# Weights split one step later in the attention, their last part loaded and split behind it, and one chunk of scores in other banks

## The chip, the cores and the metric

The kernel runs on one core of one Trainium2 chip. The time is device microseconds of one execution; the median of three is given, with the lowest and the highest. The engines are PE (TensorE, matrix products and transposes, writing to PSUM banks), ACT (ScalarE), DVE (VectorE), POOL (GpSimd) and SP (SyncE, which here only issues DMAs). Each engine works through its own instructions in the order written; between engines there are only semaphores.

## The reference

Three parts follow each other, all in float32:

```
attention  q, k, v: [4 batches, 8 heads, 576 rows, 64]
           scores = q k^T / 8, masked where 64-row block i < block j
           probs  = exp(scores - max) / (sum + 1e-9);  attn = probs v
           x = attn, heads side by side: [2304 tokens, 512]
first net  h = x w_in [512, 2048]; g = max(h, 0) + log1p(exp(-|h|)); y = g w_out [2048, 512]
experts    tokens with y w_skip > 0: expert = argmax(y w_gate) of 8,
           out = y + weight * (relu(y w1[e]) w2[e]);  other tokens: out = y
```

## The kernel before

**Attention** (`attention`, called first in each engine's program). The 32 (batch, head) pairs are taken two at a time: 16 pairs p of heads. For each p the 576 rows of scores come in five chunks i = 0 to 4 of 128 rows (the last of 64). PE multiplies a chunk (`score`, L333 and L339) into PSUM, DVE masks it and takes its negative maximum (`two_maxima` for chunks 0 and 1, `maximum` for the others), ACT takes the exponential and the sum (`exponent`, L459), DVE forms the inverse of the sums (`invert`, L574 and L575; once for chunks 0 to 2, once for 3 and 4), POOL multiplies probs by it (`scale`, L269), PE turns probs (`turn_probs`, L352, units named p0, p1, p2a, p2b, p3a, p3b, p4, p4end), ACT and DVE copy what is turned out of PSUM, and PE multiplies with v (`mix_left` L364, `mix_right` L376). The turns of probs and the mixtures of pair p are written in step p+1, between the scores of pair p+1. PE also turns q and k of the next pair (`turn_qk`: units q, k, ends; L319, L313), and DVE copies them to qT and kT (`copy_qk`).

**Banks.** PSUM has eight banks: four for scores, two for `turned`, two for `mixed`. `score_tile` gives chunks 0, 1 and 3 of a pair banks 0 and 1 of scores, chunks 2 and 4 banks 2 and 3. `score` therefore waits on the semaphore `probs_ready`, which ACT raises after each chunk's exponentials: chunk 3 for chunks 0 and 1 of its pair, chunk 4 for chunk 2, chunk 0 of the next pair for chunk 3, chunk 2 of the next pair for chunk 4. The two `turned` banks alternate: each unit waits for the copy of the unit before the last. The mixtures' first use of `mixed` is `mix_left(0)`, in step 1.

**Weights.** w_in and w_out are kept in two parts each, a rounded `high` and the remainder `low`, and every product is made of three. The split is done while the attention runs: 16 parts w of 128x1024, eight of w_in and eight of w_out. SP loads part w to one of two halves of `stage` (`load_weights`), and POOL makes high (a cast, L280) and low (a subtraction, L282) in `split(w)`. In POOL's order, step p (0 to 15) is: the scalings of chunks 3 and 4 of pair p-1, then `split(p)`, then the scalings of chunks 0 to 2 of pair p. SP loads parts 0 and 1 ahead of its loop and part p+1 in its round p, behind the loads of q, k and v of later pairs; a load waits until the part that was in its half of stage is split.

**The blocks** (`rest`). The 2304 tokens are taken in six blocks of 384, and the loop over n has its own body for the first and the last. In each block there are 16 hidden chunks f (L999 to L1001: x by columns of w_in) and 16 product rows (`rows_chunk`, L1010 to L1012: g by rows f of w_out), three chunks behind; the softplus between them is ACT's (L1221 to L1227) and DVE's (L1405 to L1411). Product rows 13 to 15 of a block lie in the round of the next block. Then ACT copies the finished rows to `y` (`copy_rows`), SP stores y, and POOL sorts rows to the experts. Hidden chunks 0 to 2 of block 0 are written between the last turns and mixtures of the attention. `x_parts`, `mag`, `u` and others of this part lie where `stage` and q and k of the attention were, and `y` where the attention's `probsT` is; so DVE's third and fourth split of x (`split_x(2)`, `split_x(3)`) wait for weights_split 15 and ACT's first softplus for 16. Last come the experts, whose weights are loaded at the end of the blocks.

The change touches `score_tile` and `score` (PE's waits and banks), SP's loop in `sync`, POOL's loop in `gpsimd`, the wait in `vector`, and in `rest` SP's, POOL's, PE's (`rows_chunk`) and ACT's (`copy_rows`) programs.

Of the kernel before, what the change touches and what calls it, by code (L numbers as in the profile page):

```python
# [25 lines left out]
P = 128  # L26
# [41 lines left out]
def build(nc, q, k, v, w_in, w_out, w_skip, w_gate, w1, w2, out):  # L68
    B, H, S, D = q.shape
    DM, FF = w_in.shape  # L70
    E, _, EF = w1.shape
    N = B * S
    PAIRS = B * H // 2
    JP = H // 2
    CH = (S + P - 1) // P
    FULL = S // P
    TAIL = S - FULL * P
    assert D == 64 and DM == H * D == 4 * P and TAIL == 64 and CH == 5
    SCALE = 1.0 / 8.0
    assert SCALE * SCALE * D == 1.0  # L80

    x_heads = nc.dram_tensor("x_heads", (DM, N), F32).ap()


    x_sorted = nc.dram_tensor("x_sorted", (E * (N + ROUND) + ROUND, DM + 2), F32).ap()

    qf, kf, vf = (t.rearrange("b h s d -> (b h) s d") for t in (q, k, v))

    whole = ExitStack()

    def sem(name, into=whole):
        return into.enter_context(nc.semaphore(name))

    def sb(into, name, shape, dtype=F32):
        return into.enter_context(nc.sbuf_tensor(name, shape, dtype))

    def ps(into, name, shape):
        return into.enter_context(nc.psum_tensor(name, shape, F32))

    with whole:  # L100
        ident = sb(whole, "ident", [P, P])
        with ExitStack() as feed:

            win = {p: sb(feed, f"w_in_{p}", [P, DM // P, FF], F32R) for p in ("high", "low")}
            wout = {p: sb(feed, f"w_out_{p}", [P, FF // P, DM], F32R) for p in ("high", "low")}
            x_raw = sb(feed, "x_raw", [P, DM // P, TILES * P])
            router = sb(feed, "router", [P, DM // P, GROUP])
            x_stored = sem("x_stored")
            attended = attention(nc, qf, kf, vf, w_in, w_out, w_gate, w_skip, x_heads, ident, win, wout, x_raw, router,
                                 x_stored, sem, sb, ps, (B, H, S, D, PAIRS, JP, CH, FULL, TAIL, SCALE, DM, FF, E))  # L110
            rest(nc, x_heads, x_sorted, out, w1, w2, ident, win, wout, x_raw, router,
                 x_stored, PAIRS, attended, feed, sem, sb, ps, (N, DM, FF, E, EF))


def attention(nc, qf, kf, vf, w_in, w_out, w_gate, w_skip, x_heads, ident, win, wout, x_raw, router,
# [3 lines left out]
    with own:  # L119
# [41 lines left out]
        SPLIT = 2 * P  # L161

# [21 lines left out]
        def score_tile(p, i):  # L186

            if i < 2:
                return scores[:, 0:2, ROW[i]:ROW[i] + P * (i + 1)]
            b = 2 if i % 2 == 0 else 0  # L190
            return scores[:, b:b + 2, 0:P * (i + 1)] if i < FULL else scores[:, b:b + 2, 0:S // 2]

        def sync(sp):
# [44 lines left out]
            load_weights(0)  # L238
            load_weights(1)
            for p in range(PAIRS + 2):  # L240
# [3 lines left out]
                if 1 < p < PAIRS:  # L244
                    load_v(p)
                if 0 < p < PAIRS - 1:
                    load_weights(p + 1)
                if p > 1:
# [12 lines left out]
        def gpsimd(pool):  # L261
# [22 lines left out]
            for p in range(PAIRS + 1):  # L284
                if p > 0:
                    pool.wait_ge(s["inverse_ready"], 2 * p)
                    for two in range(2):
                        scale(3, two)
                    scale(FULL, 0)
                if p < PAIRS:  # L290
                    split(p)
                    pool.wait_ge(s["inverse_ready"], 2 * p + 1)
# [4 lines left out]
        def tensor(pe):  # L297
# [25 lines left out]
            def score(p, i):  # L323
                if i == 0:
                    pe.wait_ge(s["copied_by_vector"], copies[p - 1, "ends"][1])

                if i != 1 and CH * p + i > 2:
                    pe.wait_ge(s["probs_ready"], CH * p + (-1, None, 0, 2, 3)[i])
                tile = score_tile(p, i)
# [210 lines left out]
        def vector(dve, split_x):  # L540
# [88 lines left out]

            dve.wait_ge(s["weights_split"], PAIRS - 1)  # L630
            split_x(2)
# [12 lines left out]

def rest(nc, x_heads, x_sorted, out, w1, w2, ident, win, wout, x_raw, router,
         x_stored, PAIRS, attended, feed, sem, sb, ps, sizes):
# [84 lines left out]
    counted = parts[0:1, 0:E * MOST[0]].rearrange("p (e m) -> p e m", e=E)  # L731

    hidden = ps(feed, "hidden", [P, 2, BANK])
    rows_out = ps(feed, "rows_out", [P, TILES, DM])
# [11 lines left out]
             "exps_ready", "chosen_ready", "ranks_ready", "slots_ready", "sorted",  # L746
             "tally_ready", "blank", "closed", "closed_by_pool", "parts_ready", "parts_copied", "constants_ready", "vector_steps", "constant_steps", "waited")
    s = {n: sem("b_" + n) for n in names}
# [41 lines left out]
    with late:  # L790
# [32 lines left out]
        def _(sp):  # L823
# [6 lines left out]
            def store_rows(n):  # L830
                sp.wait_ge(s["rows_copied"], TILES * (n + 1))
                sp.dma_start(out[bass.ds(n * T, T), :].rearrange("(t p) d -> p t d", p=P), y[:, :, 0:DM])\
                  .then_inc(s["rows_stored"], 16)

            sp.wait_ge(x_stored, 16 * PAIRS)
            sp.wait_ge(s["x_ready"], K)
# [76 lines left out]
        def _(pool):  # L913
# [28 lines left out]
                           allow_small_or_imprecise_dtypes=True).then_inc(s["constants_ready"], 1)  # L942

            def sort(n):

# [39 lines left out]
        def _(pe):  # L985
# [27 lines left out]

            def rows_chunk(n, f):
                pe.wait_ge(s["g_ready"], F * n + f + 1)
                for t in range(TILES):
# [198 lines left out]
        def _(act):  # L1215
# [19 lines left out]
            def copy_rows(n, t):  # L1235
                if t == 0:
                    act.wait_ge(x_stored, 16 * PAIRS)
                    need(act, s["rows_stored"], 16 * n)
                    need(act, s["sorted"], 16 * TILES * n)
# [41 lines left out]

            act.wait_ge(att["weights_split"], PAIRS)
            chunk(0, 0)
# [391 lines left out]
```

## Time and profile before

| | |
|---|---|
| median of 3 runs | 700.47 us (699.14 to 701.51) |
| the profiled execution | 700.94 us |
| its span, first to last instruction | 699.3 us |
| mean granted clock of PE | 0.991 of full |
| PE busy | 676.8 us (97%) |
| PE's weight loads busy | 521.2 us (75%) |
| DVE, ACT, POOL busy | 433.3 us (62%), 404.5 us (58%), 165.4 us (24%) |
| chain that ended last | PE 86%, DVE 4%, DMA 2%, issue 2%, SP's queue 2%, ACT 1%, POOL 1% |

All times below are microseconds from the span's start. The attention lasts until about 211, the blocks until about 640, the experts to the end. A row of the timeline gives the start, how long it took, the engine, the line, the operation and its tiles (out<-in), the count of like instructions merged into the row, and in brackets how long the engine was idle before it and who released it. Successive matmuls overlap at their ends, so the start of the next row says better than a row's length how long PE was held. The granted clock is given as a share of full speed: 1.00 is 2.4 GHz, 0.50 is 1.2 GHz.

### The profile page before, as it was taken

The numbers are of one execution on the slowest core, as the hardware profiler recorded it, in microseconds if no ns is written. First come the engines' busy times: TensorE is split into PE (matmuls) and PEld (weight loads), VectorE is DVE, ScalarE is ACT, GpSimd is POOL, SyncE is SP. The second block draws the span as 40 slices with busy tenths as digits, with TensorE's granted clock in tenths as the row PEclk, the third lists the DMA queues.
The fourth block names the chain that finished last, engine by engine and source line by source line (L and its number), as shares of the span: only waits on it lengthen the run. The fifth ranks groups of instructions, "written<-read, shape, count | busy, mean of one in ns | idle before, by whom it ended". The sixth has DMA issues, their size and how long they took to land.

```text
span 699.3 us, 12929 instructions
## 1 busy us (share of the span) xinstructions
PE 676.8 (97%) x3990; PEld 521.2 (75%) x3990; DVE 433.3 (62%) x1049; ACT 404.5 (58%) x990; POOL 165.4 (24%) x227
## 2 busy tenths in 40 slices
PE   6999999999999999999999999999999999999895
PEld 4565555656578999889989998899888988864342
DVE  5566676767666676567656765676567656746122
ACT  3576666667775566656565656565656565542221
POOL 2767767676741000001000200020002000103111
PEclk9899999999999999999999999999999999999998
DMA  8355665554202000200020002000200010079170
GB/s 202 92 154 140 174 169 144 148 138 125 83 35 70 1 1 1 92 0 12 0 90 0 9 0 90 0 0 0 90 0 12 0 45 0 3 260 357 52 257 25
DMA packets 79439, 53.73 MB, mean 77 GB/s; under 512 B 61192, under 2 KB 64264, under 8 KB 79392
## 3 DMA queue, kind: packets, MB, share of 16 engines
q1 hardware_dynamic: 75952, 50.60, 24.1%
q0 software_dynamic: 1920, 1.73, 0.9%
q10 hardware_dynamic: 1520, 0.82, 0.4%
q8 instruction: 24, 0.39, 0.2%
q14 instruction: 23, 0.19, 0.1%
HBM read 41.18 MB, written 16.28 MB: 82 GB/s over the span
## 4 chain that ended last, share of the span: by engine, by line
PE 86%; DVE 4%; DMA 2%; issue 2%; SPq 2%; ACT 1%; POOL 1%; DVEq 0%; ACTq 0%; POOLq 0%
PE hidden L999 9%; PE hidden L1001 9%; PE hidden L1000 9%; PE rows_out L1012 9%; PE rows_out L1010 9%; PE rows_out L1011 9%; PE turned L352 8%; PE scores L333 6%; PE mixed L376 5%; PE scores L339 2%; PE hidden L1113 2%; PE rows_out L1128 2%; PE mixed L364 2%; DMA softplus_done<-x_sorted 1%; PE turned_y L1037 1%
## 5 line engine op out<-in xcount | busy, mean ns | idle before, releaser
L1221 ACT ACTIVATE mag<-hidden 128x384 f32<-128x384 f32 x96 | 47.3, 492 | 151.6 <-PE hidden L1001 149.8
L999 PE MATMUL hidden<-x_parts,w_in_high 128*128 (+1 forms) x384 | 132.8, 346 | 0.5 <-DVEq L1413 0.4
L1001 PE MATMUL hidden<-x_parts,w_in_low 128*128 (+1 forms) x384 | 129.4, 337 | 0.0
L1000 PE MATMUL hidden<-x_parts,w_in_high 128*128 (+1 forms) x384 | 129.4, 337 | 0.0
L948 POOL DMA_INDIRECT x_sorted<-y,slot x18 | 20.5, 1140 | 406.7 <-DVE slot L1462 403.1
L1012 PE MATMUL rows_out<-w_out_high,g_low 128*128 128x512 f32 x288 | 114.0, 396 | 0.0
L1010 PE MATMUL rows_out<-w_out_high,g_high 128*128 128x512 f32 x288 | 113.7, 395 | 0.4 <-DVE g_low L1420 0.4
L1011 PE MATMUL rows_out<-w_out_low,g_high 128*128 128x512 f32 x288 | 113.5, 394 | 0.0
L459 ACT ACTIVATE probs<-scores,neg_max 128x128 f32<-128x128 f32 (+3 forms) x128 | 67.1, 530 | 21.7 <-DVE neg_max L554 15.1
L269 POOL TENSOR_SCALAR probs<-probs,inverse 128x128 f32<-128x128 f32 (+3 forms) x128 | 66.9, 544 | 52.6 <-DVE inverse L575 52.6
L999 PEld LDWEIGHTS hidden<-x_parts,w_in_high 128*128 128x128 f32 x384 | 72.1, 188 | 8.3 <-issue 3.1
L1420 DVE TENSOR_TENSOR g_low<-g,g_high 128x384 fp32r<-128x384 f32 x96 | 53.6, 558 | 36.4 <-DVE g L1411 34.3
L1000 PEld LDWEIGHTS hidden<-x_parts,w_in_high 128*128 128x128 f32 x384 | 72.2, 188 | 2.2
L1001 PEld LDWEIGHTS hidden<-x_parts,w_in_low 128*128 128x128 f32 x384 | 72.1, 188 | 0.0
L1405 DVE TENSOR_SCALAR small<-u 128x384 uint32<-128x384 f32 x96 | 34.8, 362 | 59.0 <-ACT u L1223 57.8
L1410 DVE COPY_PREDICATED log<-small,series 128x384 f32<-128x384 uint32 x96 | 58.1, 605 | 17.3 <-DVE series L1407 17.3
L1012 PEld LDWEIGHTS rows_out<-w_out_high,g_low 128*128 128x128 f32 x288 | 54.1, 188 | 12.5
L352 PEld LDWEIGHTS turned<-ident,probs 128*128 128x128 f32 x320 | 34.3, 143 | 36.9 <-issue 27.5
L1010 PEld LDWEIGHTS rows_out<-w_out_high,g_high 128*128 128x128 f32 x288 | 54.1, 188 | 9.5 <-DVE g_low L1420 1.1
L1011 PEld LDWEIGHTS rows_out<-w_out_low,g_high 128*128 128x128 f32 x288 | 54.1, 188 | 8.7
L352 PE MATMUL turned<-ident,probs 128*128 128x128 f32 x320 | 53.1, 290 | 5.2 <-ACT probsT L468 3.2
L1407 DVE SCALAR_TENSOR_TENSOR series<-square,u 128x384 f32<-128x384 f32 x96 | 53.3, 555 | 4.5
(179 smaller groups left out, 1058.0 us busy)
## 6 DMA issues: line engine op xcount, KB each, us to landing
whole_w<-in_moe_w_dram SPq DMA_DIRECT2D x12, 1024.0 KB, 11.3
x_heads<-x_pair SPq DMA_DIRECT2D x16, 288.0 KB, 2.1
x_raw<-x_heads SPq DMA_DIRECT2D x6, 768.0 KB, 5.6
out_dram<-y SPq DMA_DIRECT2D x6, 768.0 KB, 4.0
q_nat<-in_q_dram SPq DMA_DIRECT2D x32, 128.0 KB, 2.6
v_nat<-in_v_dram SPq DMA_DIRECT2D x32, 128.0 KB, 2.4
stage<-in_moe_w_in_dram SPq DMA_DIRECT2D x8, 512.0 KB, 3.9
stage<-in_moe_w_out_dram SPq DMA_DIRECT2D x8, 512.0 KB, 3.7
```

The lines of the kernel that those rows point to most:

```text
L269: nc.gpsimd.tensor_scalar(to, to, inverse[:, i, two:two + 1], 1.0, ALU.mult, ALU.mult)\
L352: last = nc.tensor.transpose(to[0:kr, n * P:n * P + P], rows[:, P * c:P * c + kr], ident[:])
L459: last = nc.scalar.activation(to, scored, ACT.Exp, bias=neg_max[:, i, two:two + 1], accum_out=sums[:, i, two:two + 1])
L999: nc.tensor.matmul(o, win["high"][:, k, cols], high, start=(k == 0), stop=False)
L1000: nc.tensor.matmul(o, win["high"][:, k, cols], low, start=False, stop=False)
L1001: last = nc.tensor.matmul(o, win["low"][:, k, cols], high, start=False, stop=(k == K - 1))
L1010: nc.tensor.matmul(o, high, wout["high"][:, f, :], start=(f == 0), stop=False)
L1011: nc.tensor.matmul(o, high, wout["low"][:, f, :], start=False, stop=False)
L1012: return nc.tensor.matmul(o, low, wout["high"][:, f, :], start=False, stop=(f == F - 1))
L1407: step.then(nc.vector.scalar_tensor_tensor(series[:], square[:, b, :], REST, u[:, b, :], ALU.add, ALU.mult))
L1410: step.then(nc.vector.copy_predicated(log[:, b, :], small[:], series[:]))
L1420: nc.vector.tensor_tensor(g_low[f % RING][:], g[:, f % 2, :], g_high[f % RING][:], ALU.subtract)\
```

## The change

There are two edits.

1. **Part w is split in step w+1.** POOL's step 0 has no split; step p has `split(p-1)` for p from 1 to 15. SP loads only part 0 ahead of its loop and part p in round p, for p from 1 to 14. Part 15, the last two rows f of w_out (14 and 15), is not split in the attention: behind the last mixture SP loads it to the place of `y`, POOL splits it behind its constants, PE waits for that ahead of product row 14 of each block but the last (a wait that is written in the loop), and ACT ahead of each block's first copy to y. DVE's x_parts 2 and 3 still wait for 15 splits, which is now the split made in step 15; ACT's first softplus waits for 15 in place of 16.
2. **The fourth chunk of scores of pair 0** goes to the two banks of `mixed` and waits for nothing; chunk 0 of pair 1 then waits only for the exponentials of chunks 0 and 1 of pair 0.

```diff
+        LAST_PART = PAIRS - 1
@@ score_tile
+            if p == 0 and i == 3:
+                return mixed[:, :, 0:P * (i + 1)]
             b = 2 if i % 2 == 0 else 0
@@ sync
             load_weights(0)
-            load_weights(1)
             for p in range(PAIRS + 2):
...
-                if 0 < p < PAIRS - 1:
-                    load_weights(p + 1)
+                if 0 < p < LAST_PART:
+                    load_weights(p)
@@ gpsimd
                     scale(FULL, 0)
+                    if p <= LAST_PART:
+                        split(p - 1)
                 if p < PAIRS:
-                    split(p)
                     pool.wait_ge(s["inverse_ready"], 2 * p + 1)
@@ score
-                if i != 1 and CH * p + i > 2:
-                    pe.wait_ge(s["probs_ready"], CH * p + (-1, None, 0, 2, 3)[i])
+                if i != 1 and CH * p + i > 2 and (p, i) != (0, 3):
+                    pe.wait_ge(s["probs_ready"], CH * p + (-1 if p > 1 else -3, None, 0, 2, 3)[i])
@@ vector
-            dve.wait_ge(s["weights_split"], PAIRS - 1)
+            dve.wait_ge(s["weights_split"], LAST_PART)
@@ rest
+    last_part = y[:].rearrange("p t d -> p (t d)")[:, 0:2 * DM]
+    LAST_F = 2 * (PAIRS - 1 - PAIRS // 2)
@@ rest, sync
+            sp.wait_ge(att["mixed_right_ready"], PAIRS)
+            sp.dma_start(last_part.rearrange("p (f n) -> p f n", n=DM),
+                         w_out[LAST_F * P:(LAST_F + 2) * P, :].rearrange("(f p) n -> p f n", p=P))\
+              .then_inc(s["last_part_loaded"], 16)
             sp.wait_ge(x_stored, 16 * PAIRS)
@@ rest, gpsimd, behind the constants
+            pool.wait_ge(s["last_part_loaded"], 16)
+            high, low = (wout[h][:, LAST_F:F, :].rearrange("p f n -> p (f n)") for h in ("high", "low"))
+            nc.gpsimd.tensor_copy(high, last_part).then_inc(s["last_part_high"], 1)
+            pool.wait_ge(s["last_part_high"], 1)
+            nc.gpsimd.tensor_tensor(low, last_part, high, ALU.subtract).then_inc(s["last_part_split"], 1)
@@ rows_chunk
+                if f == LAST_F:
+                    pe.wait_ge(s["last_part_split"], 1)
                 pe.wait_ge(s["g_ready"], F * n + f + 1)
@@ copy_rows
                     act.wait_ge(x_stored, 16 * PAIRS)
+                    act.wait_ge(s["last_part_split"], 1)
@@ scalar of rest
-            act.wait_ge(att["weights_split"], PAIRS)
+            act.wait_ge(att["weights_split"], PAIRS - 1)
```

## Rows read from the trace of the kernel before

**Rows 1.** Busy time in two stretches: length, engines (x instructions), PEclk, DMA share, GB/s
```profile
30.00:60.00 30.00, 29.33 (x223) 17.78 (x222) 19.57 (x51) 20.34 (x64) 21.97 (x32) 1.00 0.53 138
220.00:280.00 60.00, 60.00 (x303) 54.38 (x302) 39.70 (x81) 36.14 (x77) 0.00 (x0) 1.00 0.00 1
```

**Rows 2.** Timeline of PE, steps 0 and 1
```profile
8.93 0.66 PE L319 MATMUL turned<-ident,q_nat 128*128 128x128 f32 x4
11.49 1.13 PE L333 MATMUL scores<-kT,qT 64*128 64x512 f32 x4 [1.90 <-ACT probs L459]
...
13.40 1.19 PE L339 MATMUL scores<-kT,qT 64*64 64x288 f32 x8
15.78 0.93 PE L333 MATMUL scores<-kT,qT 64*128 64x128 f32 x8 [1.19 <-ACT probs L459]
18.41 0.69 PE L352 MATMUL turned<-ident,probs 128*128 128x128 f32 x2 [1.71 <-POOL probs L269]
19.32 1.11 PE L352 MATMUL turned<-ident,probs 128*128 128x128 f32 x4 [0.22 <-POOL probs L269]
...
25.72 0.66 PE L352 MATMUL turned<-ident,probs 128*128 128x128 f32 x4
```

**Rows 3.** Timeline of POOL, split of part 0 and pair 0's scalings
```profile
14.17 1.04 POOL L280 CAST w_in_high<-stage 128x1024 fp32r<-128x1024 f32 x1 [12.48 <-DMA stage<-in_moe_w_in_dram]
15.29 2.34 POOL L282 TENSOR_TENSOR w_in_low<-stage,w_in_high 128x1024 fp32r<-128x1024 f32 x1
17.62 4.10 POOL L269 TENSOR_SCALAR probs<-probs,inverse 128x128 f32<-128x128 f32 x8
```

**Rows 4.** Timeline of DVE, steps 0 and 1
```profile
10.77 0.68 DVE L595 TENSOR_SCALAR qT<-turned 128x512 f32<-128x512 f32 x1
12.72 0.17 DVE L561 MEMSET scores<- 64x128 f32 x1 [1.27 <-PE scores L333]
...
14.07 0.68 DVE L597 COPY kT<-turned 128x512 f32<-128x512 f32 x1
...
15.26 0.19 DVE L575 RECIPROCAL inverse<-sums_eps 128x6 f32<-128x6 f32 x1
```

**Rows 5.** Busy time in three stretches around the fall of the clock
```profile
8.00:12.00 4.00, 2.10 (x14) 1.08 (x12) 2.94 (x7) 2.28 (x11) 0.00 (x0) 1.00 0.77 171
14.00:18.00 4.00, 1.51 (x14) 0.63 (x10) 3.25 (x12) 2.28 (x6) 3.75 (x4) 1.00 1.05 257
18.00:25.00 7.00, 6.37 (x22) 3.86 (x24) 2.78 (x7) 3.17 (x12) 6.92 (x10) 0.52 0.50 125
```

**Rows 6.** Timeline of ACT, end of pair 0's third chunk and copy of p0
```profile
12.34 0.23 ACT L459 ACTIVATION_READ_ACCUMULATOR probs<-scores,neg_max 128x1 f32 x1
...
20.99 0.36 ACT L468 COPY probsT<-turned 128x256 f32<-128x256 f32 x1
```

**Rows 7.** Timeline of PE, third chunk of scores to p3a in step 2
```profile
34.08 0.92 PE L333 MATMUL scores<-kT,qT 64*128 64x384 f32 x4
...
37.64 0.66 PE L352 MATMUL turned<-ident,probs 128*128 128x128 f32 x4
```

**Rows 8.** Issue of q of pair 2 by SP, and its time to landing
```profile
11.28 0.98 SPq L200 DMA_DIRECT2D q_nat<-in_q_dram  x2
...
q_nat<-in_q_dram SPq DMA_DIRECT2D x2, 128.0 KB, 4.5
```

**Rows 9.** Timelines of POOL, DVE and SP at the attention's end
```profile
191.22 2.65 POOL L282 TENSOR_TENSOR w_out_low<-stage,w_out_high 128x1024 fp32r<-128x1024 f32 x1
...
195.60 0.28 DVE L587 COPY probsT<-turned 64x128 f32<-64x128 f32 x1
...
193.34 18.38 SPq L230 DMA_DIRECT2D x_heads<-x_pair  x3
```

**Rows 10.** Timeline of PE, product row 14 of block 0
```profile
271.61 0.39 PE L1010 MATMUL rows_out<-w_out_high,g_high 128*128 128x512 f32 x1
```

**Rows 11.** Waits of PE: total, times, longest
```profile
PE hidden L1113 <- issue: 1.8, 2, 1.3
```

More of the change, by code:

```diff
@@ L110, in build @@
                                  x_stored, sem, sb, ps, (B, H, S, D, PAIRS, JP, CH, FULL, TAIL, SCALE, DM, FF, E))
-            rest(nc, x_heads, x_sorted, out, w1, w2, ident, win, wout, x_raw, router,
+            rest(nc, x_heads, x_sorted, out, w_out, w1, w2, ident, win, wout, x_raw, router,
                  x_stored, PAIRS, attended, feed, sem, sb, ps, (N, DM, FF, E, EF))
@@ L642, in attention, with rest @@
     return sync, gpsimd, tensor, scalar, vector, s, turned_count
-def rest(nc, x_heads, x_sorted, out, w1, w2, ident, win, wout, x_raw, router,
+def rest(nc, x_heads, x_sorted, out, w_out, w1, w2, ident, win, wout, x_raw, router,
          x_stored, PAIRS, attended, feed, sem, sb, ps, sizes):
@@ L731, in rest @@
     counted = parts[0:1, 0:E * MOST[0]].rearrange("p (e m) -> p e m", e=E)
+    last_part = y[:].rearrange("p t d -> p (t d)")[:, 0:2 * DM]
+    LAST_F = 2 * (PAIRS - 1 - PAIRS // 2)
+    assert LAST_F == F - 2
     hidden = ps(feed, "hidden", [P, 2, BANK])
@@ L746, in rest @@
              "exps_ready", "chosen_ready", "ranks_ready", "slots_ready", "sorted",
-             "tally_ready", "blank", "closed", "closed_by_pool", "parts_ready", "parts_copied", "constants_ready", "vector_steps", "constant_steps", "waited")
+             "tally_ready", "blank", "closed", "closed_by_pool", "parts_ready", "parts_copied", "last_part_loaded", "last_part_high", "last_part_split", "constants_ready", "vector_steps", "constant_steps", "waited")
     s = {n: sem("b_" + n) for n in names}
```

## The prediction

> **What bounds the kernel now.** The page's busy shares and its chain of waits (table above) come first: PE is busy nearly throughout and is most of the chain. Then the busy time by stretches: from 30 to 60 us, in the attention, PE works 29.33 of 30 us, from 220 to 280 us, in the blocks, all 60.00 [rows 1]. So a change can win only where PE's queue is thin, and lose only by what it puts into the full part. The thin place is the beginning, and I read PE's instructions there one by one, with POOL, DVE and ACT beside them.
>
> The reader sees three gaps in PE [rows 2]: 1.90 us ahead of pair 0's fourth chunk of scores (11.49), which waits for ACT's exponentials to free its banks; 1.19 us ahead of pair 1's first scores (15.78), the same reason two chunks further; 1.71 us ahead of the first turned probs (18.41), which wait for POOL's scaling. POOL is late because the split of weight part 0 stands ahead of the scalings in its queue: it waits for its load until 14.17 and works until 17.62, though DVE has had the inverse ready at 15.26+0.19 = 15.45 [rows 3, 4]. Behind the gaps the granted clock falls: it is 1.00 (2.4 GHz) over 8-12 and 14-18 us and 0.52 on average over 18-25, which is 1.2 GHz for nearly all of it [rows 5]. Ahead of the fall, in 14-18, PE had been busy 1.51 of 4 us.
>
> **Term 1, the start of the chain.** I walk the new order with the old durations.
> PE: the turn of q of pair 1 begins at 8.93 and takes 0.6 (its row says 0.66, the last matmul overlapping). The fourth chunk goes to mixed's two banks and waits for nobody: 9.5 in place of 11.49, and with 1.1 it ends at 10.6. The turn of k, as long as that of q, ends at 11.2. The turn of the ends needs the bank that DVE empties with qT, 10.77+0.68 = 11.4, and is over by 11.8 [rows 2, 4]. The fifth chunk still waits for the third's exponentials, ACT 12.34+0.23 = 12.57 [rows 6]: 12.6 in place of 13.40. With 1.1 it ends at 13.7.
> DVE: mask and maximum of the fourth chunk took 14.07-12.72 = 1.35 and now begin behind qT at 11.4, to 12.75. kT, the ends and the inverse took 15.45-14.07 = 1.4: the ends are copied by 13.6, the inverse is ready at 14.1 [rows 4]. The masks and maxima work on mixed's banks as they did on those of scores, the same instructions of the same size.
> Pair 1's first scores want only the first two chunks' exponentials (over before 12) and the ends: they start at 13.7, not 15.78.
> POOL: with no split in step 0 it scales when the inverse is there, 14.1 and a semaphore, say 14.2, in place of 17.62. The second turn of probs came 19.32-17.62 = 1.70 behind that start, so now 15.9 [rows 2, 3]. **It is 3.4 us earlier.** What is late next is DVE's inverse; no load stands before it any more.
> Loads that must keep up: q of pair 2 is issued from 11.28 to 12.3 and lands 4.5 later, 16.8 at most [rows 8], and is wanted at 18.0 (below). SP now issues one 512 KB load less ahead of it, so it comes earlier if anything; k of pair 1 stands further ahead still. Part 0's load, there at 14.17, is wanted behind pair 0's scalings, at 14.2+4.10 = 18.3 and later.
>
> **Term 2, the clock.** From the second turn (19.32) to the turn called p3a (25.72) PE took 6.40 us, nearly all at the low rate [rows 2, 5]. At the high rate: the second turn 0.5 (half of its 1.11), to 16.4; from the third chunk to p3a a later step takes 37.64-34.08 = 3.56 [rows 7], which gives 20.0. One wait of that stretch is longer here: the third turn needs ACT's copy of the first, whose end was 20.99+0.36 = 21.35, 2.03 behind the second turn's start [rows 6]; less the 0.5 by which that turn is shorter it is 17.5, and without it the third turn would start at 16.4+0.85 = 17.3. So +0.3: p3a at 20.3, 4.4 us behind the second turn in place of 6.4. **That is 2.0 us more**, if the clock stays high. Low rate remains possible, so I weigh it by the nearest rows. In 8-12 us PE was busy 2.10 of 4 us and the clock was still high in 14-18; in 14-18 it was busy 1.51, and the clock fell [rows 5]. In the new order its gaps are 0.2 at 11.2, 0.8 at 11.8, 0.4 ahead of the first turn of probs, 0.6 between it and the second, 0.3 ahead of the third: no 4 us with less than 2.5 busy. That is nearer to the row that kept the clock. I take 2.0; the ends are 0 and 2.3 (ACT's 0.3 gone too).
> The Trainium skill (TensorE: Matmul & The Clock Gate, "The HAM clock gate") says that how many matmuls run at the low rate differs from run to run of one kernel. One profile of before stands here, so no row shows that; by it some runs of before would lose less than 2.0, and the changed kernel's time would be what the sum gives.
>
> **From p3a on** PE's order is the old one and PE has no slack to swallow the lead [rows 1], so all of it is carried on. A POOL step keeps its scalings and one split, with the part's number one less; each part is loaded one round later and used one later, with the same distance between. Cost 0, hidden by the time POOL had to spare in each step.
> **Step 15.** DVE's x_parts 2 and 3 now wait for a split of this very step. That split (now of part 14) ended at 191.22+2.65 = 193.87; DVE comes there at 195.60+0.28 = 195.8 [rows 9]. Hidden with 1.9 us to spare; without it, what is missing would go to hidden chunk 0's last products one for one.
> **The last part.** SP issues it behind its last store, in whose row the queue is free at 193.34+18.38 = 211.7; at the 4.5 us of the slow group it lands at 216.2 [rows 8, 9]. POOL has its constants first, then cast and subtract, 1.04+2.65 = 3.7 [rows 3, 9]: about 220 by the old clock of the trace. Its first reader is product row 14 of block 0 at 271.61 [rows 10]; some 50 us cover it, and ACT's copy to y, which now waits for it too, is two product rows later. Each queue it is moved past has room: in SP's stand the reload of x_raw for block 1 (used late in block 0) and the padding store, in POOL's the first sort, after block 0. Uncovered it would cost what it lasts beyond that, one for one.
> **Beside DVE.** The split now runs next to DVE's softplus. In step 15, next to busy DVE, POOL's subtract took 2.65 where part 0's took 2.34 [rows 3, 9]: both sides may lose some 0.3 us, and an equal loss on DVE meets products wanted three chunks later. Cost 0; with no cover 0.3 to 0.6.
> The Trainium skill (GPSIMD Engine Reference, "Key points") says that GpSimd shares its SBUF interfaces with VectorE and contends with some of its instructions. The rows agree with 0.31 us; by the rule, were all of it on the path, the sum would be up to 0.6 smaller.
> **Added waits.** PE gets one ahead of product row 14 of five blocks; behind it stand nine products and the next hidden chunk. It is satisfied long before. The nearest row: such waits stand ahead of every chunk in 220-280, and PE has no gap [rows 1]. 0 each. The other end is the longest gap of "issue" ahead of a matmul, 1.3 us in the expert tail [rows 11], far from it in kind. ACT's six stand in an engine with idle time in each chunk.
>
> **Sum.** The profiled execution took 700.94 us, 699.3 span and 1.6 around it. 3.4+2.0 = 5.4 less: 695.5. The median before is 700.47, 0.5 lower, inside the spread of its runs (699.14 to 701.51); that would make it 695.1 by median. I stay with 695.5 and leave the half us to the range.
>
> **Rivals.**
> 1. *The clock falls all the same*, somewhat earlier or later. For: 2.3 us of gaps remain within 5. Against: the denser order, by the two rows above. Only 3.4 is won: 697.5.
> 2. *Another wait in the gap's place*: a load of pair 1 or 2 comes late (or DVE does the inverse where it did), so POOL starts at 15.5, won 2.1 instead of 3.4, and with the longer gaps the clock is lost too: 698.8. For: landings of 4.5 us. Against: 1.2 us to spare at the tightest.
> 3. *Slower: the loop's new wait stalls PE*, at product row 14, five times. From 5.4/5 = 1.1 us each the kernel is slower than before, from 1.5 measurably; if each stall is as long as the longest of PE's gaps above, 1.90 [rows 2], it is 9.5 and the time 705.0. For: gaps of "issue" of 1.3 us exist behind waits of the tail [rows 11]. Against: PE has waits of this kind ahead of every chunk and no gap.
> 4. *It doesn't do what it says*: ACT or POOL sets the pace of a pair, and the lead is given back before the blocks. Against: PE is busy 29.33 of 30 us there. 700.5.
>
> **Chances.** Forecast 62% (its own range 694.2 to 696.4), rival 1 19%, rival 2 9%, rival 3 4%, rival 4 6%. The range, 694.2 to 698.0, holds the forecast and rival 1 with the unknown ends of the clock and of the contention. What a measurement of this kernel can't tell from no change is 0.3%, 2.1 us about 700.47. Faster (under 698.4): forecast, rival 1 and a third of 2, 84%. Same: rival 4 and the rest of 2, 12%. Slower: rival 3, 4%.
>
> **What would show it.** PE: the fourth chunk at 9.5 without a gap, pair 1's first scores at about 13.7, the second turn of probs at 15.9, p3a at 20.3, the clock at 1.00 from 8 to 30 us. POOL: first scaling at 14.2, its first split behind pair 0's scalings. x_parts 2 and 3 without a wait; the last part split some 50 us ahead of product row 14, and no gap there in any block. It is wrong if the clock is 0.50 anywhere from 9 to 30 us, if POOL is idle at 14.2, if DVE waits ahead of the inverse, if a pair takes longer than before, or if PE waits in the blocks.

## The result, and the profile after

| | before | changed |
|---|---|---|
| median | 700.99 us (699.14 to 702.99, 6 runs) | 697.14 us (696.10 to 698.19, 6 runs) |
| ratio, 95% interval | | 0.9942 (0.9922 to 0.9961) |
| profiled execution, span | 700.94, 699.3 us | 697.28, 695.7 us |
| mean granted clock of PE | 0.991 | 0.998 |

The changed kernel is 3.9 us faster by the medians and 3.7 by the two profiled executions; 695.5 was forecast, 5.4 less. The interval of the ratio runs from 2.7 to 5.5 us. (The ratios of this document are worked out apart from the medians and differ from their quotients by up to 0.002, so some gains are given by both.)

PE of the changed kernel, steps 0 and 1 (columns as in [rows 2]):

```profile
8.44 1.57 PE L338 MATMUL scores<-kT,qT 64*128 64x128 f32 x12 [0.46 <-DVE kT L605]
9.94 0.66 PE L324 MATMUL turned<-ident,q_nat 128*128 128x128 f32 x4
10.53 1.13 PE L338 MATMUL mixed<-kT,qT 64*128 64x512 f32 x4
11.59 0.65 PE L324 MATMUL turned<-ident,k_nat 128*128 128x128 f32 x4
...
13.62 1.19 PE L344 MATMUL scores<-kT,qT 64*64 64x288 f32 x8 [0.70 <-ACT probs L464]
14.82 0.93 PE L338 MATMUL scores<-kT,qT 64*128 64x128 f32 x8
15.96 0.44 PE L357 MATMUL turned<-ident,probs 128*128 128x128 f32 x2 [0.21 <-POOL probs L273]
16.87 0.66 PE L357 MATMUL turned<-ident,probs 128*128 128x128 f32 x4 [0.47 <-POOL probs L273]
17.45 0.92 PE L338 MATMUL scores<-kT,qT 64*128 64x384 f32 x4
18.77 0.52 PE L357 MATMUL turned<-ident,probs 128*128 128x128 f32 x3 [0.41 <-ACT probsT L473]
...
21.46 0.66 PE L357 MATMUL turned<-ident,probs 128*128 128x128 f32 x4
```

The three large gaps of [rows 2] are gone. The fourth chunk follows the turn of q with no gap, and p3a comes at 21.46 in place of 25.72: 4.26 us earlier. POOL and DVE of the same stretch:

```profile
15.17 4.09 POOL L273 TENSOR_SCALAR probs<-probs,inverse 128x128 f32<-128x128 f32 x8 [13.49 <-DVE inverse L580]
...
19.94 1.03 POOL L284 CAST w_in_high<-stage 128x1024 fp32r<-128x1024 f32 x1
```

```profile
14.68 0.16 DVE L579 TENSOR_SCALAR sums_eps<-sums 128x6 f32<-128x6 f32 x1
14.88 0.19 DVE L580 RECIPROCAL inverse<-sums_eps 128x6 f32<-128x6 f32 x1
```

POOL scales 0.1 us behind the inverse, and its first split stands behind pair 0's scalings. Against [rows 3] the scalings start 2.45 us earlier. The busy times in the stretches of [rows 5]:

```profile
8.00:12.00 4.00, 3.56 (x24) 2.05 (x24) 2.86 (x10) 1.27 (x7) 0.00 (x0) 1.00 0.75 162
14.00:18.00 4.00, 3.31 (x26) 1.64 (x22) 3.78 (x13) 3.11 (x11) 2.83 (x7) 1.00 0.72 165
18.00:25.00 7.00, 6.37 (x48) 3.78 (x44) 5.07 (x11) 5.33 (x16) 5.32 (x5) 1.00 0.42 124
```

PE is busy the same 6.37 us of the last stretch, but with 48 matmuls in it and not 22: the granted clock is 1.00 there and not 0.52. The last part, and its first reader:

```profile
211.47 1.28 POOL L960 CAST w_out_high<-y 128x1024 fp32r<-128x1024 f32 x1 [0.60 <-DMA y<-in_moe_w_out_dram]
212.84 2.83 POOL L962 TENSOR_TENSOR w_out_low<-y,w_out_high 128x1024 fp32r<-128x1024 f32 x1
```

```profile
267.37 0.39 PE L1030 MATMUL rows_out<-w_out_high,g_high 128*128 128x512 f32 x1
```

It is ready at 215.7 and wanted at 267.37, 51.7 us later. From 20 to 620 us the waits of PE (total, times, longest) are:

```profile
PE turned L357 <- ACT probsT L473: 3.4, 15, 0.3
PE hidden L1019 <- DVEq L1436: 0.5, 1, 0.5
PE rows_out L1030 <- DVE g_low L1443: 0.4, 1, 0.4
```

The kernel before has the same three kinds (3.2, 0.4 and 0.4 us). The last two lie in the last block, which has no wait for the last part: the third is ahead of its product row 14, at 615.46, and waits for DVE's g_low. At product row 14 of the five blocks that do wait for the last part PE has no gap. Comparing matmul by matmul, the lead of 4.26 us at p3a is 4.25 at the end of the attention and 4.33 late in the last block. The tail of experts is 0.7 longer here: from the 3500th of 3990 matmuls to the end of the span took 90.7 us before and 91.4 after.

### The profile page after: what moved, and what is told of

Read it like the earlier page. It is cut to its first block, busy times and chain, and to the rows that moved or that the text cites. A ratio compares the mean times of both kernels' runs of the same rounds, so it can differ in the third digit from the quotient of the medians.

```text
span 695.7 us, 12935 instructions
## 1 busy us (share of the span) xinstructions
PE 675.2 (97%) x3990; PEld 520.5 (75%) x3990; DVE 434.6 (62%) x1049; ACT 404.2 (58%) x990; POOL 165.7 (24%) x227
## 4 chain that ended last, share of the span: by engine, by line
PE 90%; DVE 4%; issue 2%; ACT 2%; DMA 1%; POOL 0%; DVEq 0%; ACTq 0%; POOLq 0%
PE hidden L1019 9%; PE hidden L1021 9%; PE hidden L1020 9%; PE rows_out L1032 9%; PE rows_out L1030 9%; PE rows_out L1031 9%; PE turned L357 8%; PE scores L338 6%; PE mixed L381 5%; PE rows_out L1150 3%; PE hidden L1135 3%; PE scores L344 3%; PE mixed L369 2%; PE turned_y L1059 1%; ACT probsT L473 1%
## 5 line engine op out<-in xcount | busy, mean ns | idle before, releaser
L464 ACT ACTIVATE probs<-scores,neg_max 128x128 f32<-128x128 f32 (+3 forms) x126 | 65.6, 527 | 18.7 <-DVE neg_max L559 16.5
L1433 DVE COPY_PREDICATED log<-small,series 128x384 f32<-128x384 uint32 x96 | 58.2, 607 | 17.3 <-DVE series L1430 17.3
L357 PE MATMUL turned<-ident,probs 128*128 128x128 f32 x320 | 51.7, 285 | 4.5 <-ACT probsT L473 3.9
```

What stands on the lines that cost most here:

```text
L357: last = nc.tensor.transpose(to[0:kr, n * P:n * P + P], rows[:, P * c:P * c + kr], ident[:])
L464: last = nc.scalar.activation(to, scored, ACT.Exp, bias=neg_max[:, i, two:two + 1], accum_out=sums[:, i, two:two + 1])
L1433: step.then(nc.vector.copy_predicated(log[:, b, :], small[:], series[:]))
```

## Experiments

The table has, of every profile, the start of pair 0's first scores, POOL's first scaling and p3a, then p3a behind the first scores and behind the scaling, the stretch from the 100th to the 3500th matmul, and the tail behind it (filler matmuls not counted in the numbering). All are worked out from starts in the traces.

| kernel | first scores | POOL scales | p3a | scores to p3a | scaling to p3a | 100th to 3500th | tail | low clock between 10 and 690 us |
|---|---|---|---|---|---|---|---|---|
| before | 7.43 | 17.62 | 25.72 | 18.29 | 8.10 | 582.2 | 90.7 | 18.2, for 6.8 |
| banks_only | 8.12 | 17.31 | 24.39 | 16.27 | 7.08 | 582.2 | 93.2 | 19.7 and 644.3, for 3.4 each |
| weights_only | 8.50 | 16.48 | 23.75 | 15.25 | 7.27 | 582.1 | 91.6 | 13.9, for 3.4 |
| filled | 8.12 | 18.24 | 26.30 | 18.18 | 8.06 | 582.1 | 92.0 | 12.8, for 3.4 |
| filled_to_fit | 8.37 | 17.57 | 23.85 | 15.48 | 6.28 | 582.1 | 91.4 | 651.7, for 3.4 |
| before_late | 8.67 | 17.64 | 25.86 | 17.19 | 8.22 | 582.1 | 91.7 | 18.5, for 6.8 |
| changed | 8.44 | 15.17 | 21.46 | 13.02 | 6.29 | 582.1 | 91.4 | none |
| changed_again | 8.68 | 15.41 | 21.70 | 13.02 | 6.29 | 582.2 | 90.5 | none |
| after_late | 9.30 | 16.03 | 22.32 | 13.02 | 6.29 | 582.2 | 93.2 | 651.3, for 3.4 |
| two_splits | 7.90 | 14.63 | 20.92 | 13.02 | 6.29 | 584.0 | 91.8 | none |
| hoisted | 8.04 | 14.77 | 21.06 | 13.02 | 6.29 | 582.2 | 91.4 | none |
| inverse_first | 8.69 | 14.56 | 22.67 | 13.98 | 8.11 | 582.4 | 90.8 | 21.2, for 3.4 |
| load_first | 8.05 | 14.78 | 21.07 | 13.02 | 6.29 | 582.0 | 91.0 | none |

The times, each beside the kernel before on the same chip:

| kernel | median us | before there | ratio (95%) |
|---|---|---|---|
| banks_only | 701.58 | 701.13 | 1.0006 (0.9989 to 1.0023) |
| weights_only | 699.62 | 701.13 | 0.9977 (0.9963 to 0.9991) |
| filled | 702.24 | 701.13 | 1.0018 (1.0002 to 1.0035) |
| two_splits | 699.07 | 701.13 | 0.9990 (0.9973 to 1.0007) |
| filled_to_fit | 699.47 | 699.21 | 1.0000 (0.9991 to 1.0010) |
| hoisted | 696.53 | 699.21 | 0.9961 (0.9946 to 0.9975) |
| inverse_first | 696.98 | 699.21 | 0.9964 (0.9950 to 0.9978) |
| before_late | 701.12 | 699.32 | 1.0011 (0.9995 to 1.0028) |
| after_late | 697.87 | 699.32 | 0.9978 (0.9968 to 0.9988) |
| load_first | 696.49 | 699.32 | 0.9956 (0.9938 to 0.9973) |
| changed_again | 696.71 | 699.32 | 0.9958 (0.9943 to 0.9972) |

**banks_only.** The kernel before with the second edit alone.

```diff
+            if p == 0 and i == 3:
+                return mixed[:, :, 0:P * (i + 1)]
...
-                if i != 1 and CH * p + i > 2:
+                if i != 1 and CH * p + i > 2 and (p, i) != (0, 3):
-                    pe.wait_ge(s["probs_ready"], CH * p + (-1, None, 0, 2, 3)[i])
+                    pe.wait_ge(s["probs_ready"], CH * p + (-1 if p > 1 else -3, None, 0, 2, 3)[i])
```

> Only the fourth chunk of scores of pair 0 goes to mixed's banks; the weights are loaded and split as before. My theory: POOL's split of part 0 (it ends at 17.62 in the profile of before) holds the scalings, so PE's turns of probs stay at 18.4 and 19.3 and the time stays within 0.5 us of the kernel before, 700.5 to 701; the gap only moves from ahead of the fourth chunk to behind pair 1's scores (which start near 14 instead of 15.78). The rival, that the banks are what binds the start, expects 2 us less or more: 699 or under.

Measured 701.58 us, no difference clear of the noise. The gap moved as expected; PE:

```profile
14.50 0.93 PE L335 MATMUL scores<-kT,qT 64*128 64x128 f32 x8
18.11 0.44 PE L354 MATMUL turned<-ident,probs 128*128 128x128 f32 x2 [2.68 <-POOL probs L271]
```

Pair 1's scores are 1.28 us earlier than in [rows 2], and the turn behind them waits 2.68 us for POOL. So the new banks alone are worth nothing that could be measured: the split holds the scalings.

**weights_only.** The first edit alone: the changed kernel without the two lines of `score_tile` and with the old wait in `score`.

```diff
-            if p == 0 and i == 3:
-                return mixed[:, :, 0:P * (i + 1)]
...
-                if i != 1 and CH * p + i > 2 and (p, i) != (0, 3):
-                    pe.wait_ge(s["probs_ready"], CH * p + (-1 if p > 1 else -3, None, 0, 2, 3)[i])
+                if i != 1 and CH * p + i > 2:
+                    pe.wait_ge(s["probs_ready"], CH * p + (-1, None, 0, 2, 3)[i])
```

> Only the weights are moved (one step later, last part behind the last mixture); the banks of scores stay as before. My theory: the inverse is there at 15.45, POOL scales from 15.6, PE's first turn of probs waits for pair 1's scores (16.7), the second for POOL, 17.3 in place of 19.32: 2.0 us less by that. The clock: PE's gaps of 1.9 and 1.2 us stay, the one of 1.7 goes; if the clock stays high from 18 to 25 us, 2.0 more. 697 with a high clock, 699 with a fall of it. The rival, that the banks do all of it, expects the time of before.

1.6 us faster by the ratio, near the smaller of the two expected gains (699 with a fall of the clock), and its profile has such a fall, from 13.9. There are two limits on POOL's first scaling. The split of part 0 ends at 17.3 to 17.6 in the profiles of before and banks_only, whenever PE starts. DVE's inverse lets POOL begin 7.98 us behind the first scores with the old banks, and 6.73 with the new ones. The first edit takes the split away, the second brings the inverse forward by 1.25 us, which shows only once the split is gone. So the pair is worth more than the sum of the two alone (0 and 1.6 here, against 2.9 and 4.1 for both); these times come from different chips, and the changed kernel was not run on this one.

**filled.** PE's gaps in the kernel before filled with products that nobody reads.

```diff
+            def fill(count):
+                for _ in range(count):
+                    nc.tensor.matmul(mixed[:, 0, 0:P], ident[:], ident[:], start=True, stop=True)
...
+                if p == 1:
+                    fill(6)
                 score(p, 0)
                 score(p, 1)
+                if p == 1:
+                    fill(10)
```

> The kernel before, with 6 matmuls of ident by ident ahead of pair 1's first scores and 10 behind its second chunk, into mixed's first bank, which is unused until then; they fill the gaps in which PE waits. Nothing comes earlier. My theory of the second term: the clock does not fall between 18 and 25 us, so p3a comes at about 23.7 instead of 25.7, and the time is 2.0 us under the kernel before, 698.8. The rival (the stretch from 19.3 to 25.7 is slow for another reason than the clock, waits on POOL or ACT) expects the time of before.

702.24 us, slower by 1.3 by the ratio, whose interval only just excludes no change. The expectation failed for two reasons that the trace shows. The fillers were too long:

```profile
16.74 1.60 PE L389 MATMUL mixed<-ident 128*128 128x128 f32 x12
18.27 0.93 PE L333 MATMUL scores<-kT,qT 64*128 64x128 f32 x8
19.13 2.50 PE L389 MATMUL mixed<-ident 128*128 128x128 f32 x20
```

They held pair 1's scores until 18.27 and the turn behind them until 21.46. And the clock fell all the same, at 12.8, behind the one gap left empty (10.3 to 12.19). As a test of the clock it is inconclusive.

**filled_to_fit.** As `filled`, with 4 and 6 in place of 6 and 10, and a third place:

```diff
+                if p == 0:
+                    fill(7)
                 score(p, 3)
```

> The kernel before, with matmuls of ident by ident into mixed's first bank, fitted to PE's gaps: 7 ahead of pair 0's fourth chunk, 4 ahead of pair 1's first scores, 6 behind its second chunk (0.12 us each by the earlier filled kernel, whose 6 and 10 held PE itself up). Measured from pair 0's first scores to the turn p3a of step 1, the kernel before took 18.3 us with the clock at 0.50 from 18 to 25 us. If the second term is right, no fall of the clock and 16.2 to 16.5 us, and a time about 1.5 to 2 us under the kernel before (699 to 699.5). If the low clock is not what made that stretch long, 18.3 and the time of before.

The trace says yes, the time no. From the first scores to p3a it took 15.48 us, less than the 16.2 expected, because the first scores came at 8.37 and the scalings did not move. POOL scales at 17.57, where it did before (17.62), and p3a comes at 23.85 and not 25.72; the clock is 1.00:

```profile
18.00:25.00 7.00, 6.38 (x45) 4.21 (x45) 5.35 (x13) 5.37 (x18) 6.92 (x10) 1.00 0.46 120
```

From scaling to p3a it took 6.28 us, as in the changed kernel (6.29), against 8.10: the fall of the clock cost **1.82 us** in the profile of before. But the median is that of the kernel before on this chip. The likely reason is that there that kernel lost less than in its profile, which no profile of it from this chip shows: its 15 runs have clocks of 0.993 to 0.998 and a median of 699.21. On the chip of the first four experiments, its 16 runs with a clock of 0.993 or less took 700.6 to 703.3 us, all but one of them over 701.1, the 15 above that 699.4 to 701.6, all but two of them under 700.2. By the traces a fall of 6.8 us lowers the mean clock by 6.8*0.5/699 = 0.005, about what lies between these two groups. The clock does not settle it alone: on the chip of the last four runs, the kernel before took, at 0.993 and 0.994, anything from 698.7 to 701.2 us. Another thing moves the kernel before from run to run as well: POOL could begin part 0's cast at 13.74 to 14.41 in the five profiles with the old load order and a split in step 0.

**two_splits.** The changed kernel with the last part in `stage` and split in step 15.

```diff
                 if 0 < p < LAST_PART:
                     load_weights(p)
+                if p == LAST_PART - 1:
+                    load_weights(LAST_PART)
...
                     if p <= LAST_PART:
                         split(p - 1)
+                    if p == LAST_PART:
+                        split(LAST_PART)
...
-            pool.wait_ge(s["last_part_loaded"], 16)
...
-                if f == LAST_F:
-                    pe.wait_ge(s["last_part_split"], 1)
...
-            act.wait_ge(att["weights_split"], PAIRS - 1)
+            act.wait_ge(att["weights_split"], PAIRS)
```

> The changed kernel, but the last part stays in the attention: loaded to stage in round 14, and POOL splits parts 14 and 15 one after the other in step 15, ahead of pair 15's scalings; no new waits in the blocks. My theory: POOL had 1.0 us idle there, the second split takes 3.7, so the scalings of pair 15 come 2.7 us late, PE's turns behind hidden chunk 0 wait for them (1.5 to 2.7 us), and the time is 1.5 to 2.7 us above the changed kernel. If PE has other work ahead of these turns that hides it (hidden chunk 0, 2.4 us), under 0.5 us above. If the added waits in the blocks cost something, this kernel gives it back and is less slow than that, or faster.

The stretch from the 100th to the 3500th matmul is 1.9 us longer than in the changed kernel, and the median is about 2 us above that of the changed kernel (on another chip). POOL and PE at that place:

```profile
190.17 2.38 POOL L288 TENSOR_TENSOR w_out_low<-stage,w_out_high 128x1024 fp32r<-128x1024 f32 x1
192.52 5.27 POOL L275 TENSOR_SCALAR probs<-probs,inverse 128x128 f32<-128x128 f32 x8
```

```profile
193.01 0.44 PE L1013 MATMUL hidden<-x_parts,w_in_high 128*128 128x384 f32 x1 [1.16 <-DVE x_parts L1411]
194.90 0.66 PE L361 MATMUL turned<-ident,probs 128*128 128x128 f32 x4 [0.35 <-POOL probs L275]
```

PE waits 1.16 us for DVE's x_parts and 0.35 for the scalings. The size came out as expected, but for the most part by another way than the late scalings. DVE's two instructions for x_parts, here and in the changed kernel:

```profile
191.09 2.34 DVE L1411 TENSOR_TENSOR x_parts<-x_raw,x_parts 128x384 fp32r<-128x384 f32 x2
```

```profile
191.54 1.12 DVE L1420 TENSOR_TENSOR x_parts<-x_raw,x_parts 128x384 fp32r<-128x384 f32 x2
```

The first of the two took 1.87 us beside POOL's second subtraction (190.17 to 192.55), 0.65 in the changed kernel. Sending the last part behind the attention is therefore worth 1.9 us, once the splits have moved.

**hoisted.** The changed kernel, its waits for the last part ahead of the loops.

```diff
-                if f == LAST_F:
-                    pe.wait_ge(s["last_part_split"], 1)
...
+            pe.wait_ge(s["last_part_split"], 1)
             with pe.Fori(1, BLOCKS) as n:
...
-                    act.wait_ge(s["last_part_split"], 1)
...
+            act.wait_ge(s["last_part_split"], 1)
             with act.Fori(1, BLOCKS - 1) as n:
```

> The changed kernel with the waits for the last part taken out of the loops: PE waits once ahead of its loop over blocks, ACT once ahead of its own. If the five waits of PE and six of ACT cost anything, the stretch from p3a to the end of the blocks (582.1 us in the profiles of before and changed alike) gets shorter; my theory is that it stays within 0.1 us and the time is that of the changed kernel, 697.1, within 0.5. The changed kernel's tail behind matmul 3500 was 91.4 us to 90.7 of before, in one profile each; if the added instructions in the loops did that, it comes back to 90.7 here.

582.15 us against 582.11 and 582.17 in the two profiles of the changed kernel: the waits cost nothing. The tail did not come back (91.4). The median, 696.53, is 0.6 under the 697.1 expected, on another chip.

**inverse_first.** `hoisted`, with DVE's order changed in step 0.

```diff
                 maximum(p, 3)
+                if p == 0:
+                    invert(p, False)
                 if load:
                     copy_qk(p + 1, "k")
...
-                invert(p, False)
+                if p > 0:
+                    invert(p, False)
                 maximum(p, 4)
```

> The kernel with the hoisted waits, and in step 0 DVE forms the first inverse ahead of the copies of k and ends of pair 1. In the changed kernel POOL's first scaling waited for this inverse (15.17, 6.7 us behind pair 0's first scores). If the inverse is what is late now, POOL starts 0.7 us earlier, the second turn 0.4 us earlier, and the time is 0.4 under the hoisted kernel. The rival: DVE as a whole is the bound of these steps, pair 1's scores start 0.5 later for it, p3a comes no earlier, and the time is the same or up to 0.3 more.

The rival is right. POOL scales 5.87 us behind the first scores instead of 6.73, but PE:

```profile
15.34 0.93 PE L338 MATMUL scores<-kT,qT 64*128 64x128 f32 x8 [0.27 <-DVE kT L605]
...
19.30 0.52 PE L357 MATMUL turned<-ident,probs 128*128 128x128 f32 x3 [1.38 <-ACT probsT L473]
```

The third turn waits 1.38 us for ACT, whose exponentials wait for DVE's maxima; it starts 10.61 us behind the first scores, in `hoisted` 10.33. Behind it this profile even has a fall of the clock (21.2). The median is 0.45 above `hoisted`, inside the intervals.

**before_late and after_late.** In each of the two kernels

```diff
-WARM_FIRST = 9
+WARM_FIRST = 14
```

> The kernel before with 14 instead of 9 warm-up products, so PE comes about 1 us later (1.0 to 1.9) to pair 0's first scores. My theory: in the kernel before, POOL's first scaling is tied to the load of weight part 0 (17.3 to 17.6 in the profiles of before and banks_only, though the first scores began at 7.4 and 8.1), so a late PE costs nothing until DVE's inverse passes that point, 1.4 us later: the time is less than 0.7 us above the kernel before, apart from what the clock does. The rival (the start of PE moves everything in both kernels) expects 1.0 to 1.9 us more.

> The changed kernel with the same 14 warm-up products. My theory: here POOL's first scaling follows DVE's inverse, 6.7 us behind pair 0's first scores in every profile so far, so what PE is late shifts everything: 1.0 to 1.9 us above the changed kernel, and the gain over the kernel with the late start before it is about 1 us smaller than the gain without. The rival expects the same addition in both kernels.

The first scores of before_late came at 8.67, 1.24 us later than in the profile of before, and POOL's first scaling at 17.64 and p3a at 25.86 stood where they were (17.62, 25.72). Its POOL and DVE:

```profile
13.82 1.04 POOL L280 CAST w_in_high<-stage 128x1024 fp32r<-128x1024 f32 x1 [12.14 <-DMA stage<-in_moe_w_in_dram]
14.94 2.34 POOL L282 TENSOR_TENSOR w_in_low<-stage,w_in_high 128x1024 fp32r<-128x1024 f32 x1
17.64 4.09 POOL L269 TENSOR_SCALAR probs<-probs,inverse 128x128 f32<-128x128 f32 x8 [0.36 <-DVE inverse L575]
```

```profile
16.17 1.15 DVE L574 TENSOR_SCALAR sums_eps<-sums 128x6 f32<-128x6 f32 x1
17.35 0.19 DVE L575 RECIPROCAL inverse<-sums_eps 128x6 f32<-128x6 f32 x1
```

The split holds POOL's start by a second way too. `sums_eps`, the step ahead of the inverse, takes 0.16 us in the changed kernel. Here it began beside POOL's subtraction, took 1.15 and ended at 17.32, the subtraction at 17.28. In `filled_to_fit` (1.38 us) and `filled` (1.97) the two ends lie within 0.03 us of each other as well. So even an inverse that could have been there before the split's end comes just behind it, and the scalings start 0.36 us behind the split; in the profile of before the inverse had come first. Part 0's load was 0.35 us earlier here than in that profile, which is why the two starts agree so closely.

In after_late the first scores came at 9.30 and p3a again 13.02 us behind them. So by the traces my theory holds: the kernel before is tied to a load and its split, the changed one to PE's start. The times do not decide it. after_late is 1.2 us above changed_again, as expected. before_late is 1.8 above the kernel before by the medians, which is what the rival expected, and 0.8 by the ratio, whose interval reaches from 0.3 below to 2.0 above. The gain with the late start should have been about 1 us smaller than without: it was 2.3 against 2.9 by the ratios, but 3.3 against 2.6 by the medians.

**load_first.** The kernel before with the new banks and one load issued sooner; no part is moved.

```diff
+            load_weights(0)
             sp.wait_ge(s["zeros_ready"], 1)
             load_v(0)
             load_v(1)
-            load_weights(0)
             load_weights(1)
```

> The kernel before with the new banks, and SP issues the load of weight part 0 ahead of the loads of v for pairs 0 and 1; the splits stay where they were and there is no separate last part. If what held the start is the arrival of part 0 in front of the scalings, POOL has split it by about 14.4 (issue at 6.5, 4 to landing, 3.5 of work), as early as DVE's inverse comes, and the time is within 0.5 us of the changed kernel on the same chip. If it is the split as such, or its DMA holding up the loads of q and k, it stays at least 1.5 us above the changed kernel.

696.49 us, against 696.71 for changed_again on the same chip. Its POOL:

```profile
10.11 1.04 POOL L282 CAST w_in_high<-stage 128x1024 fp32r<-128x1024 f32 x1 [8.43 <-DMA stage<-in_moe_w_in_dram]
11.23 2.35 POOL L284 TENSOR_TENSOR w_in_low<-stage,w_in_high 128x1024 fp32r<-128x1024 f32 x1
14.78 4.10 POOL L271 TENSOR_SCALAR probs<-probs,inverse 128x128 f32<-128x128 f32 x8 [1.20 <-DVE inverse L577]
```

The split ends 1.2 us before the inverse comes, and all that follows is the changed kernel's, to 0.01 us (13.02, 6.29). Part 0's load was issued at 6.48 here and at 10.17 in the kernel before. So it was the late load in front of the split, by the order of SP's queue, that held the start; the split itself, once loaded early, is hidden. load_first ties the changed kernel and needs neither the last part's own path nor its waits.

**changed_again.** The changed kernel itself.

> The changed kernel unchanged, on the same chip as the other three, to compare them: 696.5 to 697.5. Its first scores and the rise of the clock ahead of them should lie elsewhere than in its first profile (8.44 and 6.8), with POOL's first scaling 6.7 us behind the first scores and p3a 6.3 behind that again.

As expected: 696.71 us, the clock rose at 7.5, the first scores came at 8.68, POOL's first scaling 6.73 and p3a 13.02 behind them. Its tail took 90.5 us, so the 91.4 of the first profile need not be the change's doing.

## Why the prediction was right, and where it was off

**Term 1, the walk.** The forecast put POOL's first scaling 14.2-7.43 = 6.8 us behind pair 0's first scores and p3a 20.3-7.43 = 12.9 behind them. Measured: 6.73 and 13.02, in all six profiles in which no split stands in the way and DVE's order is the old one (changed, changed_again, after_late, two_splits, hoisted, load_first). DVE was late next, as said: `inverse_first` shows that its whole load, with ACT's behind it, bounds these steps, not the inverse alone.

**Its size.** What failed is the point from which I walked. I took 7.43, the start of the first scores in one profile, as given in both kernels; over the eleven profiles with 9 warm-up products it lies between 7.43 and 8.69, and the profile of before had the earliest. In the traces the kernel before does not care, up to 8.67 (before_late), and the changed one passes it on in full (after_late). So the 3.4 us were 2.45 between the two profiles, 1.0 of it missing because the changed kernel's profile had its first scores at 8.44. That is the larger part of what lies between 695.5 and the profiled 697.28; 0.2 is term 2, the rest the tail. So the step that failed is the pricing of the load that no longer stands in the way: it had been hiding how late PE starts.

**The range.** 697.14 lies outside the forecast's own 694.2 to 696.4. It lies inside 694.2 to 698.0 only because that range was stretched to hold rival 1, which did not come; that part is luck. Two of the prediction's own signs of being wrong also came: POOL was idle at 14.2, until 15.17, and PE waits in the last block. The first is the later start of PE, since no load and no other work of DVE than forecast stood in between, so rival 2 did not come either. The second is there in the kernel before too.

**Term 2, the clock.** Forecast 2.0, measured 1.82 between profiles (`filled_to_fit`, and the changed kernel's 6.29 to 8.10). The prediction rounded up on the way: its third turn comes at 15.9+2.03-0.5 = 17.43 against 17.25, which is +0.2 and not +0.3. The clock stayed at 1.00 from its rise up to p3a in all six; rival 1 did not come. What one profile could not show is whether the kernel before pays this in every run. Its mean clock ranges from 0.988 to 0.997 over 31 runs on one chip, with the times in two groups, and `filled_to_fit` removes 1.8 us from the trace and nothing from the median on a chip where before's runs have the higher clocks. That speaks against it, but no profile of before without the fall was taken. The Trainium skill (TensorE: Matmul & The Clock Gate, "The HAM clock gate") has the number of matmuls at the low rate at a kernel's start differ between runs of one kernel. The traces agree for the start: in the two profiles of the changed kernel the clock rose at 6.8 and at 7.5 us. The gain of the changed kernel is 4.1 us by the ratio in the first comparison and 2.9 in that of changed_again, as it would be if the kernel before loses less on the chip of the second; that is argued, not shown.

**From p3a on.** All of the lead was carried, 582.1 against 582.2 us; rival 4 did not come.

**Step 15** had room: x_parts ran at 191.54 behind a split that ended at 186.95+2.65 = 189.60, 1.9 us as forecast.

**The last part.** 51.7 us of cover, 50 forecast. **Added waits**: 0 by `hoisted`; rival 3 did not come.

**Beside DVE** the size was wrong, and the cover held. I put 0.3 to 0.6 us on the contention, from a subtraction of 2.65 us in step 15 against 2.34 for part 0. These rows don't show contention with a busy DVE, for beside part 0's DVE was busy too, 3.25 of 4 us [rows 5]. The runs show it elsewhere, and larger. While POOL subtracts the last part, DVE's `small` takes 1.62 us instead of 0.36:

```profile
214.27 1.62 DVE L1428 TENSOR_SCALAR small<-u 128x384 uint32<-128x384 f32 x1 [0.87 <-ACT u L1245]
```

That is 1.26 us on one softplus, and no matmul waits for it. In the start, which the prediction didn't look at for this, the same kind of neighbour held `sums_eps` for up to 1.97 us (before_late, `filled_to_fit`, `filled`), and in `two_splits` it cost PE most of what it lost.

**The tail** was taken as fixed. It took 90.5 to 92.0 us in the ten profiles with no fall of the clock in it, and 91.4 to 93.2 in three that have one at 644 to 652; by changed_again its length need not belong to the change. Its 0.7 us is the rest of what lies between the forecast and the profiled time.

## What to carry to other kernels

A chain can be tied to a load or to an engine's start, and removing the load moves it to the other: before sizing the gain, look at how far the new anchor moves from run to run, since one profile of before may show it at its best. Two edits must be judged together when one moves a limit that the other uncovers: alone they were worth 0 and 1.6 us, together 3 to 4. And when work is in front of something urgent in a queue, try issuing its load earlier before moving the work: here that did as much, with less.

## What the runs showed of the hardware

- The start of PE's real work follows the moment at which the granted clock first rises, which differs from profile to profile with the same 9 warm-up products (and between the two of the changed kernel, 6.8 and 7.5): rise at 4.6 us, first scores at 7.43 (before); 5.9 and 8.05 (load_first); 6.8 and 8.44 (changed); 7.5 and 8.68 (changed_again). Between the first and the last of these, 1.25 of 2.9 us reach the scores.
- Between 10 and 690 us the clock fell for 3.4 us at a time, for 6.8 us, or not at all. The fall of 6.8 in the profile of before cost 1.8 us (8.10 against 6.28 from scaling to p3a). It came behind gaps of PE of at most 1.90 us each.
- Four DVE instructions took much longer beside a POOL subtraction of 128x1024: `small` 1.62 us for 0.36 (changed; the subtraction itself 2.83, elsewhere 2.34 to 2.66), `sums_eps` 1.15, 1.38 and 1.97 for 0.16 (before_late, `filled_to_fit`, `filled`). The three `sums_eps` ended within 0.04 us of the subtraction's end.
